# Sums and low parts of x on GpSimd, block-product copy ahead of roundings, finer waits for the parts of g, in an attention, routing and gated-product kernel

## What is computed

```python
def _moe_ref(x, w_gate, w1, w2):
    ...                                   # assign 192 of 1536 tokens to each of 8 experts
    for e in range(E):
        mask = assigned == e
        h = np.maximum(x[mask] @ w1[e], 0.0)      # 512 -> 1024
        out[mask] = h @ w2[e]                     # 1024 -> 512
    return out

def _moe2_ref(x, w_a, w_b, w_out):
    a = x @ w_a                                   # 512 -> 1536
    b = x @ w_b
    return (a * b @ w_out)                        # 1536 -> 512
```

## Time and profile before

| | us |
|---|---|
| three timed runs | 720.5, 726.58, 729.08 |
| median | 726.58 |
| the profiled execution, its own time | 722.27 |
| its span from first to last instruction | 720.1 |

### The profile page before, as it was taken

How to read it: one execution, slowest core, us unless ns; L and a number is a source line. 1 busy time by engine, 2 the same in 40 slices (tenths; PEclk the granted TensorE clock), 3 DMA queues, 4 the chain that set the end, 5 groups by cost and what they waited for, 6 DMA issues and landing times.

```text
span 720.1 us, 10960 instructions
## 1 busy us (share of the span) xinstructions
PE 626.4 (87%) x3840; PEld 557.2 (77%) x3840; DVE 458.4 (64%) x1148; ACT 319.7 (44%) x804; POOL 274.0 (38%) x283
## 2 busy tenths in 40 slices
PE   7999999996429999988895997897989999999994
PEld 4877777765228999988795986787888888988893
DVE  3677567744753777777874477877756455546553
ACT  3676567642304777655555242242323334233310
POOL 4000000000024221212228776663846788777623
PEclk8999999996558999999998999998989999999999
DMA  9953150404014576745640221201212141210002
GB/s 191 263 120 88 32 161 24 139 24 139 0 35 144 177 234 221 230 151 178 215 147 30 69 78 45 74 30 58 59 33 85 59 144 61 89 30 30 29 1 87
DMA packets 87511, 72.06 MB, mean 100 GB/s; under 512 B 39840, under 2 KB 74656, under 8 KB 87456
## 3 DMA queue, kind: packets, MB, share of 16 engines
q1 hardware_dynamic: 85536, 65.05, 30.8%
q0 software_dynamic: 1920, 6.29, 2.6%
HBM read 65.04 MB, written 6.29 MB: 99 GB/s over the span
## 4 chain that ended last, share of the span: by engine, by line
PE 68%; DVE 20%; ACT 6%; issue 3%; DMA 1%; POOL 0%; DVEq 0%; ACTq 0%; POOLq 0%
PE psum L1747 11%; PE psum L1825 7%; PE psum L1827 6%; PE psum L1828 6%; PE psum L1560 5%; PE psum L1748 5%; PE psum L1740 5%; PE psum L1742 5%; PE psum L1741 5%; PE psum L1538 3%; PE psum L1525 3%; PE psum L1565 2%; DVE t_tmp L1361 2%; PE psum L1502 2%; ACT above L832 2%
## 5 line engine op out<-in xcount | busy, mean ns | idle before, releaser
L673 POOL TENSOR_TENSOR w_lo<-w_raw,w_hi 128x512 fp32r<-128x512 f32 x96 | 109.5, 1173 | 60.5 <-ACT w_hi L865 57.9
L1747 PE MATMUL psum<-h_hl,w_hi 128*128 128x384 f32 x256 | 82.9, 389 | 13.1 <-DVE h_hl L1399 13.1
L1825 PE MATMUL psum<-t_first,w_hi 128*128 128x384 f32 x168 | 61.1, 363 | 23.0 <-DVE w_raw L1445 12.8
L625 POOL TENSOR_TENSOR w_lo<-w_raw,w_hi 128x2048 fp32r<-128x2048 f32 x7 | 32.2, 4603 | 119.9 <-ACT w_hi L755 119.9
L1747 PE MATMUL psum<-x_hl,w_hi 128*128 128x384 f32 x256 | 75.4, 366 | 1.6 <-DVE x_hl L1346 1.6
L1827 PE MATMUL psum<-x_hl,w_hi 128*128 128x384 f32 x216 | 75.8, 351 | 0.0
L755 ACT ACTIVATE w_hi<-w_raw 128x1024 fp32r<-128x1024 f32 (+1 forms) x72 | 69.0, 958 | 0.0
L1748 PE MATMUL psum<-h_hl,w_lo 128*128 128x192 f32 x256 | 67.3, 263 | 0.0
L1748 PE MATMUL psum<-x_hl,w_lo 128*128 128x192 f32 x256 | 64.8, 253 | 0.0
L1825 PE MATMUL psum<-x_hl,w_hi 128*128 128x384 f32 x168 | 56.8, 338 | 8.5 <-ACT w_raw L930 8.5
L943 ACT ACTIVATE g<-psum 128x384 fp32r<-128x384 f32 x48 | 23.6, 492 | 91.4 <-DVE psum L1448 37.3
(11 more groups left out here) (220 smaller groups left out, 1609.7 us busy)
## 6 DMA issues: line engine op xcount, KB each, us to landing
w_raw<-in_moe_w_dram SPq DMA_DIRECT2D x32, 1024.0 KB, 5.5
w_raw<-in_moe_w_a_dram SPq DMA_DIRECT2D x12, 512.0 KB, 3.5
w_raw<-in_moe_w_b_dram SPq DMA_DIRECT2D x12, 512.0 KB, 3.6
w_raw<-in_moe_w_out_dram SPq DMA_DIRECT2D x12, 512.0 KB, 3.3
k_raw<-in_k_dram SPq DMA_DIRECT2D x16, 192.0 KB, 3.8
q_raw<-in_q_dram SPq DMA_DIRECT2D x16, 192.0 KB, 4.1
v_sb<-in_v_dram SPq DMA_DIRECT2D x16, 192.0 KB, 4.3
xs_scratch<-x_rows SPq DMA_DIRECT2D x8, 384.0 KB, 3.7
```

Of the source, the lines that this page charges most:

```text
L673: return nc.gpsimd.tensor_tensor(out_t, t, hi_t.bitcast(f32), ALU.subtract)
L1747: nc.tensor.matmul(bk[:, 0:2 * CAP], lhs_hi, rhs_both, start=first, stop=False)
L1825: nc.tensor.matmul(o, w_h, t_hi[:, t, :], start=(first and t == 0), stop=False, skip_group_check=True)
```

## The change

It has three parts. First, `add_t` and `split_t` move from DVE to POOL, and are spread anew. For c = 0 the four pieces lie in experts 4, 5, 6 and 6 again (none in expert 7); `round_t` on ACT moves behind group (2, 1) of an expert, the fourth piece behind (3, 1) of expert 6. For c = 1 the sums of a piece stand at the end of POOL's stages 1 to 4 and its low parts in stages 2 to 5, `round_t` in stages 2 to 5. In expert 7 ACT's first roundings of the weights of the gated product move back by two to three groups. Second, on ACT `keep_p1(0, n)` moves to the front of the stage, ahead of the last `round_g` of the stage before and of `round_mix(1, n, 0)`; DVE's low part of the last part of g moves behind its first sum of the next stage. Third, `down` waits for three of the four parts of g, and for the fourth at its fourth tile.

```diff
 # POOL
-            with pool.Fori(1, E) as e:
+            def add_t(c, q):
...
+            def split_t(c, q):
...
+            with pool.Fori(1, 4) as e:
                 split_lo(e, 3)
+            for e in range(4, E):
+                if e < E - 1:
+                    add_t(0, e - 4)
+                split_lo(e, 3)
+                if e < E - 1:
+                    split_t(0, e - 4)
+                if e == E - 2:
+                    add_t(0, 3)
+                    split_t(0, 3)
...
                 split_mix(1, n)
+                if 2 <= n <= 5:
+                    split_t(1, n - 2)
...
                     split_out(n)
+                if 1 <= n <= 4:
+                    add_t(1, n - 1)
 # ACT, experts
-                        if e >= 4 and (u, g) == (2, 0):
+                        if 4 <= e < E - 1 and (u, g) == (2, 1):
                             round_t(0, e - 4)
-                        if last and (u, g) in ((1, 0), (1, 1)):
-                            round_mix(0, 0, g)
+                        if e == E - 2 and (u, g) == (3, 1):
+                            round_t(0, 3)
+                        if last and (u, g) == (2, 0):
+                            round_mix(0, 0, 0)
                         if last and (u, g) == (2, 1):
+                            round_mix(0, 0, 1)
+                        if last and (u, g) == (3, 0):
                             round_mix(1, 0, 0)
 # ACT, stages
-                if n > 0:
-                    round_mix(1, n, 0)
                 keep_p1(0, n)
                 if n > 0:
+                    round_g(n - 1, 3)
+                    round_mix(1, n, 0)
+                keep_a11(n)
+                if n > 0:
                     round_mix(1, n, 1)
-                keep_a11(n)
+                if 2 <= n <= 5:
+                    round_t(1, n - 2)
...
-                for part in range(4):
+                for part in range(3):
                     round_g(n, part)
+            round_g(STAGES - 1, 3)
 # DVE
                 nc.vector.tensor_tensor(u2_sb, yb, p1_sb, ALU.add).then_inc(a_made, 1)
+                if n > 0:
+                    lower_b(n - 1, 3)
...
                 factor_a(n)
-                if 1 <= n <= 4:
-                    add_t(1, n - 1)
                 if n > 0:
                     keep_down(n - 1)
-                if 1 <= n <= 4:
-                    split_t(1, n - 1)
                 factor_b(n)
 # PE
-                pe.wait_ge(g_split, 4 * (n + 1))
                 pe.wait_ge(unit_lo[2], n + 1)
                 for st in range(TILES_C):
+                    if st % (TILES_C // 2) == 0:
+                        pe.wait_ge(g_split, 4 * n + (4 if st else 3))
```

More of the change, by code:

```diff
@@ L644, in _ @@
                     in_offset=bass.IndirectOffsetOnAxis(ap=ids[:, st:st + 1], axis=0)).then_inc(xg_in[st], 16)
-            with pool.Fori(1, E) as e:
-                split_lo(e, 3)
+            def add_t(c, q):
+                src = t_sources(c, q)
+                k = 4 * c + q
+                if q == 0:
+                    pool.wait_ge(grp_done, 8 * 4 * (c + 1))
+                if k > 0:
+                    pool.wait_ge(t_split, k)
+                nc.gpsimd.tensor_tensor(src[T1], src["B12"], src[B11], ALU.subtract).then_inc(t_sums, 1)
+                nc.gpsimd.tensor_tensor(src[T3], src[B22], src["B12"], ALU.subtract).then_inc(t_sums, 1)
+                pool.wait_ge(t_sums, 4 * k + 1)
+                nc.gpsimd.tensor_tensor(src[T2], src[B22], src[T1], ALU.subtract).then_inc(t_sums, 1)
+                pool.wait_ge(t_sums, 4 * k + 3)
+                nc.gpsimd.tensor_tensor(src[T4], src[B21], src[T2], ALU.subtract).then_inc(t_sums, 1)
+            def split_t(c, q):
+                src = t_sources(c, q)
+                pool.wait_ge(t_rounded, 4 * c + q + 1)
+                for (b, lo), (_, hi) in zip(t_moves(c, q, 1), t_moves(c, q, 0)):
+                    op = nc.gpsimd.tensor_tensor(lo, src[b], hi.bitcast(f32), ALU.subtract)
+                op.then_inc(t_split, 1)
+            with pool.Fori(1, 4) as e:
+                split_lo(e, 3)
+            for e in range(4, E):
[7 more added lines that the diff above has]
+                    split_t(0, 3)
             def add_blocks(u, n):
@@ L1402, in expert @@
                             split_lo(e + 1, half // 2, half % 2)
-                        if e >= 4 and (u, g) == (0, 1):
-                            add_t(0, e - 4)
-                        if e >= 4 and (u, g) == (3, 0):
-                            split_t(0, e - 4)
             for e in range(E):
@@ L1413, in made, with lower_b @@
                 return (sem_of, per * n + at)
+            def lower_b(n, part):
+                bk, f, half = G_PARTS[part]
+                dve.wait_ge(g_rounded, 4 * n + part + 1)
+                nc.vector.tensor_tensor(g_part(f, half, 1), factor_bank(1, bk), g_part(f, half, 0).bitcast(f32),
+                                        ALU.subtract).then_inc(g_split, 1)
             def factor_a(n):
@@ L1434, in factor_b @@
                 x, yb, zb, w = (factor_bank(1, at) for at in (BX, BY, BZ, BW))
-                def lower(part):
-                    bk, f, half = G_PARTS[part]
-                    dve.wait_ge(g_rounded, 4 * n + part + 1)
-                    nc.vector.tensor_tensor(g_part(f, half, 1), factor_bank(1, bk), g_part(f, half, 0).bitcast(f32),
-                                            ALU.subtract).then_inc(g_split, 1)
                 dve.wait_ge(products_b, 7 * n + P6)
@@ L1450, in factor_b @@
                 nc.vector.tensor_tensor(u3_sb, yb, p1_sb, ALU.add).then_inc(b_made, 1)
-                lower(0)
+                lower_b(n, 0)
                 dve.wait_ge(products_b, 7 * n + P5)
@@ L1460, in factor_b @@
                 nc.vector.tensor_tensor(yb, yb, a_of[21], ALU.mult).then_inc(b_made, 1)
-                lower(1)
+                lower_b(n, 1)
                 dve.wait_ge(products_b, 7 * n + P3)
@@ L1465, in factor_b @@
                 nc.vector.tensor_tensor(zb, zb, a_of[12], ALU.mult).then_inc(b_made, 1)
-                lower(2)
-                lower(3)
+                lower_b(n, 2)
             def keep_down(n):
```

22 lines of the change are left out of this document (1 added, 21 removed).

## The result

The changed kernel takes 672.86 us (median of four runs, 670.63 to 673.95) against 723.54 for the kernel before beside it (four runs, 720.26 to 729.08): a ratio of 0.929, with an interval of 0.921 to 0.936. The forecast was 672. One of the four runs of experiment 3 (683.33 us, granted clock 0.924 where the others have 0.946) was in a slower state and is left out where times are compared.

What follows compares the result with a forecast made beforehand. PE was taken as the bound wherever it is not kept waiting; savings 13.6 + 1.2 + 19.7 + 15.5 + 0.6 = 50.6 from the profiled 722.27 gave 671.7, stated as 672 us, range 665 to 685.

Steps and rivals of the forecast that it cites:

- Experts 4 to 6: With the pieces of x off DVE, these experts return to 18.20 us each: 14.1 saved, 0.5 kept back, 13.6.
- no DVE instruction beyond 1.3 us: Sign of being right: in experts 4 to 6 no DVE instruction takes longer than 1.3 us.
- The seam: Start of expert 7 to stage 1: POOL's chain of pieces adds waits, yet 44.7 us for 45.93, 1.2 saved.
- Rival (b): DVE and POOL block each other; five more meetings in the seam's chain, 6.1 for 1.2: 677 us; chance 0.11.
- Stages 1 to 4 and the copy: Stages 1 to 4 fall to stage 5's period, 19.7 saved; copy of P1 put first ends eleven 1.41 us waits, 15.5.
- POOL's fullness: Stages 2 to 4: POOL busy 23.4 us against a period of 23.06; 1 us taken for what fails.
- PE does wait for the copy of P1: The sign forecast the opposite: no wait of PE for ACT's copy of P1 in stages 1 to 11.
- POOL is idle for less than 0.5 us: Sign of being wrong: POOL idle for less than 0.5 us in stages 3 and 4.
- Rival (a): POOL becomes the bound at 0.74 us per instruction: 6.7 in place of 1 in stages 2 to 4; 681 us; chance 0.14.
- The price on POOL: A POOL instruction of 192 elements takes 0.57 us, so a piece of eleven costs 6.3 us (3.7 to 8.1).
- rival c: Stages: the wait for P1's copy becomes one for DVE's first sum at P7, 1.1 of 1.41 staying; 684 us; chance 0.08.
- The end: Last `down` waits for one low part of g and not two in a row: 0.6 us saved.

Runs made afterwards that it cites:

- experiment 3: Changed kernel with DVE's low part of the last part of g ahead of its first sum of the next stage; 674.26 us, ratio 0.933.
- experiment 8: Changed kernel with DVE's low parts of weights for experts 5 to 7 cut from 1024 to 16 columns, computation left out; 669.45 us, one run.
- experiment 9: Against experiment 6: low parts of three y blocks per c = 1 piece moved on POOL to stages 0, 1 and 5; 657.88 us, ratio 0.911.
- experiment 7: Changed kernel with the four sums of each c = 1 piece back on DVE, behind its additions of `down`; 682.67 us, ratio 0.947.
- experiment 1: Kernel before with only the copy of P1 put first in ACT's stage, pieces of x staying on DVE; 706.94 us, ratio 0.972.
- experiment 2: Changed kernel with its second and third part undone, so only the pieces of x move to POOL; 687.46 us, ratio 0.948.
- experiment 6: Against experiment 5: expert 7's first weight roundings one group earlier, stage 0's copy of P1 ahead of second block-sum rounding and `round_out`; 663.18 us, ratio 0.918.
- experiment 4: Changed kernel with the roundings of the first three pieces of x behind group (1, 1), not (2, 1); 673.64 us, ratio 0.925.
- experiment 5: Changed kernel with the four c = 0 pieces one expert earlier, one each in experts 3 to 6; 665.00 us, ratio 0.921.

## Why the prediction was right, point by point

**Experts 4 to 6: right.** Forecast 14.1 less 0.5, measured 13.0. The 0.5 kept for meetings was not needed, and the 1.1 that is missing from 14.1 is no wait, since PE is full in both windows: in the changed kernel's execution expert 3, which the change does not touch, also takes 18.56 us and not 18.20, three times 0.36 (see the last section). The sign "no DVE instruction beyond 1.3 us" was wrong: one of 2.71 and one of 1.64 stand in each of experts 5 and 6, one of 1.46 in expert 4. They cost PE nothing that shows: it is full in all three, with up to three groups of slack.

**The seam: the mechanism right, the size off.** Forecast a gain of 1.2, measured a loss of 0.2. The chain that the prediction went through is there link by link, but each link is later:

| us from the start of expert 7 | forecast | measured |
|---|---|---|
| POOL, low parts of the third piece done | 3.4 | 5.2 |
| ACT, roundings of the fourth piece done | 7.7 | 9.6 |
| POOL, unit 3 done | 16.3 | 19.1 |
| `mix(0, 0)` starts | 23.7 | 26.6 |
| P2 starts | 29.3 | 32.2 |

ACT's wait before the fourth piece is 5.64 us, and I had said 3 to 4. These rows of ACT show it in the changed kernel:

```profile
356.60 1.06 ACT L790 ACTIVATE w_hi<-w_raw 128x1024 fp32r<-128x1024 f32 x1
363.30 0.87 ACT L923 ACTIVATE t_first<-y 128x192 fp32r<-128x192 f32 x3 [5.64 <-POOL t_tmp L658]
364.08 1.11 ACT L923 ACTIVATE t_first<-t_tmp 128x192 fp32r<-128x192 f32 x4
365.09 0.47 ACT L936 ACTIVATE grp_sb<-psum 128x384 f32<-128x384 f32 x1
```

Everything behind it, the group copies first, stands until 365.09. The term that was mis-sized is the meeting of DVE and POOL: 1.2 us for one, and it was three of 1.0 (1.9 on the third piece, 0.9 on the fourth), as experiment 8 shows by taking them away. Rival (b) had the mechanism right, and its five meetings of 1.22 were too many. That experts 4 to 6 would take the delay in their three groups of slack held: PE waits nowhere in them.

**Stages 1 to 4 and the copy: the sum right, two terms off against each other.** Forecast 19.7 + 15.5 = 35.2, measured 1.5 + 26.3 + 8.6 = 36.4. The copy of P1 saves 1.69 per stage. The 1.41 of its row is the idle time from the modelled end of the last matmul to the start of the next. But matmuls overlap: before, they start every 0.172 us and last 0.34. Without the wait P2 would have started 0.17 after 557.18, so the wait costs from start to start 1.75 - 0.17 = 1.58, and the first matmul behind it takes 0.11 longer (0.44 for 0.33): 1.69. Experiment 3 shows 0.30 on top of another wait (0.23 became 0.53). Over eleven stages that is 18.6 where I had 15.5.

POOL's fullness was taken at 1 us and cost 1.9, in three periods; 0.9 more were lost in the fourth long period, which the prediction had no term for and which is not POOL's fullness (last section). Together that is 2.7 for 1. The place is the one that the prediction named as tight: ACT, POOL's sums, their rounding, `round_out`, the copy of P1 of `mix(1, n)`. In stage 4 of the changed kernel:

```profile
486.13 1.16 ACT L904 ACTIVATE w_hi<-w_raw 128x512 fp32r<-128x512 f32 x2 [7.19 <-POOL w_raw L695]
487.19 1.04 ACT L913 ACTIVATE o_hi<-w_raw 128x1024 fp32r<-128x1024 f32 x1
488.13 0.47 ACT L969 ACTIVATE w_raw<-psum 128x384 f32<-128x384 f32 x1
```

and PE there:

```profile
488.65 0.45 PE L1838 MATMUL psum<-t_first,w_hi 128*128 128x384 f32 x1 [0.45 <-ACT w_raw L969]
```

The copy waits behind two roundings for POOL's block sums, and PE waits for the copy. I had a margin of 0.2 us (17.3 for 17.5) and a POOL that falls behind by 0.3 per stage; by stage 3 the margin was used up. Two of the signs that I gave came out against me here: PE does wait for the copy of P1, 0.45 in stage 4 and 0.42 in stage 5, and POOL is idle for less than 0.5 us (busy for 22.97 of 23.20 us in the third period and 23.29 of 23.53 in the fourth). Rival (a), POOL as the bound, was thus true in part: for three periods, at 1.9 us and not 6.7. Experiment 9 takes the load away and the loss with it.

**The price on POOL: right.** 0.57 us was forecast for 192 elements; in stages the instructions start every 0.56 us and last 0.60. Rival (a) needed 0.74 and falls. The estimate of 0.42 from the 2.6 cycles per element in the Trainium skill (GPSIMD Engine Reference, section 3.1) is too low: the line through 0.74 us at 256 elements and 4.61 at 2048 leaves 0.19 us that do not shrink with the size.

**No wait at P7 (rival c): right.** No row of PE's waits names DVE's first sum in stages 1 to 11. The one row of 0.60 is for its second, before P4 in stage 7. Experiment 3 shows how near it is: one low part of 0.55 us ahead of the sum is enough.

**The end: right**, 18.56 to 17.95, 0.61.

So the 672 is right with errors that partly cancel, and that it came within 1 us is luck to that extent. From the forecast sum: 50.6 + 3.1 (the copy) - 0.9 (POOL's fullness) - 0.9 (the fourth long period) - 1.4 (the seam) - 0.6 (experts 4 to 6) - 2.2 (up to expert 4, untouched) + 0.3 (the tail) = 48.0, as between the two spans.

## What to carry to other kernels

Price a wait of TensorE from the start of the last matmul before it to the start of the first behind it, less one step, and add what the first one takes longer: here 1.69 for a row of 1.41. A longer wait can cost clock on top: in experiment 7 one of 2.58 us made the period 4.1 to 4.4 us longer. When work moves to an engine that shares its way to SBUF with another, walk its new chain with the other engine's two-input instructions laid over it, and count one full meeting for each; it only matters where the chain decides, here at the seam and, in experiment 7, ahead of one sum of DVE. An engine that is just full in three stages wants its movable work a stage or two away (here 1.9 us of periods), and a step that stands twice on the way to a deadline wants to be begun an expert earlier (7 us).

## What the runs showed of the hardware that was not expected

**Two paces of the same matmuls at full clock.** In the kernel before, and in experiments 1 to 3, 6, 8 and 9, an undisturbed expert takes 18.20 us, and a pair of its matmuls (384 and 192 columns) starts every 0.285 us. In the changed kernel and in experiments 4, 5 and 7 it is 18.56, with every second pair 0.01 us longer, at a granted clock of 1.00 in both, and in expert 3 with the same instructions. The stages show no such difference. (An expert is 64 such pairs.) Expert 2 takes 19.73 us in these executions and 19.53 in the others. Over experts 3 to 6 this is 1.4 us. What sets it is open; no edit explains it, and one profiled execution of each kernel can't tell whether it goes with the kernel or with the execution.

**A meeting costs POOL about 1.0 us and DVE what is left of POOL's instruction.** A DVE instruction of 1.22 us holds POOL for nearly its whole length. DVE waits for what is left of one POOL instruction: 4.02 for 0.34 us against one of 4.6, about 1.1 us each against those of 128x512 in experiment 7, but at most 0.4 us against those of 192 elements in experiment 8 (1.25, 1.35 and 1.64 for 1.22). Short instructions on POOL are thus the milder neighbours.

**Finished products that were counted late.** The fourth long period, 23.66, holds PE's wait of 0.60 for DVE's second sum in stage 7. That sum waits for P7, whose last matmul starts at 544.27 and takes 0.33, and ACT's copy of a11 waits for P2, whose last matmul starts at 543.23. Both engines were free by 543.6:

```profile
545.56 0.49 ACT L975 ACTIVATE a_hi<-psum 128x384 f32<-128x384 f32 x1 [2.04 <-PE psum L1841]
545.64 0.56 DVE L1447 TENSOR_TENSOR w_raw<-psum,w_raw 128x384 f32<-128x384 f32 x1 [2.05 <-PE psum L1841]
```

One stage later the same two start without such a delay:

```profile
567.26 0.49 ACT L975 ACTIVATE a_hi<-psum 128x384 f32<-128x384 f32 x1
568.30 0.56 DVE L1447 TENSOR_TENSOR w_raw<-psum,w_raw 128x384 f32<-128x384 f32 x1 [1.06 <-PE psum L1841]
```

So two engines learned some 2 and 1 us late that PE had finished. The period at this place is long in the changed kernel and in experiments 1 and 3 to 8 (23.66 to 24.33), also where POOL has no piece of x, and in experiment 9 it is not (22.79); experiment 2, where PE waits for the copy anyway, can't tell. POOL issues the six stores of the first half's rows just before, but it does so in experiment 9 too. The cause is open.
